# Tile 2's scores one step later, half of VectorE's score work behind the gate, VectorE's weight behind the powers, layer two's odd rows later

## The reference

```python
for t in range(S):                      # recurrence
    m_new = np.maximum(f_gate[:, :, t] + m, i_gate[:, :, t])
    f_stab = np.exp(f_gate[:, :, t] + m - m_new)
    i_stab = np.exp(i_gate[:, :, t] - m_new)
    C = f_stab * C + i_stab * outer(v_t, k_t)
    n = f_stab * n + i_stab * k_t
    y_t = sigmoid(o_gate_t) * (C @ q_t) / np.maximum(np.abs(n @ q_t), 1.0)
xn = x / np.sqrt(np.mean(x * x, axis=-1, keepdims=True) + 1e-06) * rms_g   # layer one
g = xn @ w_gate
x1 = (g * sigmoid(g) * (xn @ w_val)) @ w_out
h = x1 @ w_in                                                              # layer two
out = np.maximum(0.01 * h, h) @ w_out2
```

## Time and profile before

| | us |
|---|---|
| median of 3 runs | 453.7 (451.58 to 454.03) |
| the profiled execution | 453.02 |
| its span | 451.2 |
| TensorE busy | 428.3, 95% of the span |
| VectorE busy | 233.6, 52% |
| ScalarE busy | 196.0, 43% |
| GpSimd busy | 91.3, 20% |
| granted TensorE clock, mean | 0.989 of 2.4 GHz |

### The profile page before, as it was taken

How to read it: one execution, slowest core, us unless ns; L and a number is a source line. 1 busy time by engine, 2 the same in 40 slices (tenths; PEclk the granted TensorE clock), 3 DMA queues, 4 the chain that set the end, 5 groups by cost and what they waited for, 6 DMA issues and landing times.

```text
span 451.2 us, 8148 instructions
## 1 busy us (share of the span) xinstructions
PE 428.3 (95%) x3202; PEld 377.0 (84%) x3202; DVE 233.6 (52%) x439; ACT 196.0 (43%) x431; POOL 91.3 (20%) x92
## 2 busy tenths in 40 slices
PE   2768999899999999999999999999999999999997
PEld 1658998899888888888888888899999999999996
DVE  7754767567648565554633435533343433444534
ACT  1873775356527344323433225454343343333332
POOL 1473974222111111100433101440000000000000
PEclk9986999999999999999999999999999999999999
DMA  6886381333303050000222200410000000010101
GB/s 181 288 278 203 125 267 50 121 122 121 103 20 92 30 172 1 0 1 0 65 64 65 64 0 4 127 34 0 1 0 1 0 2 0 1 58 1 58 1 58
DMA packets 10756, 31.37 MB, mean 70 GB/s; under 512 B 1328, under 2 KB 3088, under 8 KB 10720
## 3 DMA queue, kind: packets, MB, share of 16 engines
q1 hardware_dynamic: 10720, 30.87, 21.2%
HBM read 28.85 MB, written 2.02 MB: 68 GB/s over the span
## 4 chain that ended last, share of the span: by engine, by line
PE 82%; issue 6%; POOL 4%; ACT 3%; DVE 2%; DMA 2%; POOLq 0%; DVEq 0%; ACTq 0%
PE gate_ps L1017 23%; PE value_ps L1017 23%; PE out_ps L1054 9%; PE out_ps L1090 9%; PE turn_ps L1090 6%; PE out_ps L1058 3%; PE c_ps L1090 3%; PE turn_ps L992 2%; POOL w_sb L422 2%; PE turn_ps L953 2%; ACT expo L485 1%; PE turn_ps L970 1%; DMA expo<-decay_scratch 1%; POOL ms L399 1%; POOL expo L391 1%
## 5 line engine op out<-in xcount | busy, mean ns | idle before, releaser
L1017 PE MATMUL gate_ps<-x_hi,w_sb 128*128 128x512 f32 (+1 forms) x280 | 69.0, 369 | 3.8 <-DVE act_buf L800 2.3
L1017 PE MATMUL value_ps<-x_hi,w_sb 128*128 128x512 f32 (+1 forms) x280 | 69.7, 372 | 0.0
L558 ACT ACTIVATE h_hi<-hid 128x512 fp32r<-128x512 f32 (+1 forms) x46 | 24.7, 537 | 76.2 <-DVE hid L806 76.1
L1017 PEld LDWEIGHTS gate_ps<-x_hi,w_sb 128*128 128x128 f32 x280 | 47.4, 191 | 12.3 <-issue 2.7
L1017 PEld LDWEIGHTS value_ps<-x_hi,w_sb 128*128 128x128 f32 x280 | 47.7, 193 | 6.2
L825 DVE TENSOR_TENSOR h_lo<-hid,h_hi 128x512 fp32r<-128x512 f32 x48 | 33.2, 693 | 33.7 <-ACT h_hi L563 33.7
L800 DVE SCALAR_TENSOR_TENSOR act_buf<-act_buf,gate_ps 128x512 f32<-128x512 f32 (+1 forms) x46 | 26.1, 568 | 46.6 <-ACT act_buf L544 46.6
L1054 PE MATMUL out_ps<-h_hi,w_sb 128*128 128x512 f32 (+1 forms) x184 | 47.8, 346 | 0.0
L563 ACT ACTIVATE h_hi<-hid 128x512 fp32r<-128x512 f32 x48 | 30.3, 632 | 38.3 <-DVE hid L813 37.2
L544 ACT ACTIVATE act_buf<-gate_ps 128x512 f32<-128x512 f32 (+1 forms) x46 | 23.0, 500 | 48.4 <-PE gate_ps L1017 48.2
L820 DVE TENSOR_TENSOR h_lo<-hid,h_hi 128x512 fp32r<-128x512 f32 (+1 forms) x46 | 32.5, 708 | 22.1 <-ACT h_hi L558 21.8
(11 more groups left out here) (140 smaller groups left out, 774.0 us busy)
## 6 DMA issues: line engine op xcount, KB each, us to landing
raw<-in_w SPq DMA_DIRECT2D x12, 544.0 KB, 4.5
expo<-decay_scratch SPq DMA_DIRECT2D x12, 512.0 KB, 5.4
att_sb<-in_tok SPq DMA_DIRECT2D x12, 484.0 KB, 4.7
raw<-in_w SPq DMA_DIRECT2D x16, 352.0 KB, 3.0
att_sb<-in_qk SPq DMA_DIRECT2D x24, 160.0 KB
out_y<-y_acc SPq DMA_DIRECT2D x12, 160.0 KB, 1.9
consts_sb<-in_consts SPq DMA_DIRECT2D x1, 129.5 KB, 2.3
gates_sb<-in_gates SPq DMA_DIRECT2D x1, 96.0 KB, 2.4
```

What stands on the lines that cost most here:

```text
L558: nc.scalar.activation(h_hi[:, r, cols], hid[:, r, 0:width(s)], ACT.Copy).then_inc(hi_done, 1)
L1017: last = nc.tensor.matmul(ps[:, 0:n], lhs, rhs, start=(j == 0), stop=(j == len(xs) - 1))
```

## The change

1. `BESIDE` changes for tiles 2, 3 and 4. Tile 2: S, R and O one step later. Tile 3: T one step earlier. Tile 4: R and O one step earlier. With that tile 2 and tile 3 become "at once".
2. VectorE does `scores(n, 1)` behind `gated(s)` in place of ahead of it.
3. The high part of tile 0 (`x_high(0)`) moves from ScalarE to VectorE as `first_x_high`, with a semaphore of its own; both first_state calls stand ahead of it. VectorE's `lo_first` of weight block 1 moves behind x_low(1).
4. ScalarE does `high1(0)` ahead of hi_weights(3), and only half of tile 2's decays ahead of step 1; the rest comes behind tanh(1).
5. GpSimd: weigh_keys(3) ahead of inverse_rms(2), and fade_state(4) ahead of lo_weights(11).
6. In layer two `x2_odd(2)` moves from behind step 47 to behind step 53, and the loop is cut in two there.

```diff
-BESIDE = {2: (0, 1, 2, 4), 3: (3, 5, 6, 8), 4: (7, 9, 10, 11), 5: (10, 12, 13, 14), 6: (14, 15, 16, 17),
+BESIDE = {2: (1, 2, 3, 4), 3: (3, 5, 6, 7), 4: (7, 8, 9, 11), 5: (10, 12, 13, 14), 6: (14, 15, 16, 17),
...
             lo_weights(5)
+            weigh_keys(3)
             inverse_rms(2)
-            weigh_keys(3)
             lo_weights(6)
...
             exponents(5)
+            fade_state(4)
             lo_weights(11)
-            fade_state(4)
...
             square(1)
-            x_high(0)
             normalise(1)
             x_high(1)
             hi_weights(2)
             first1(0, width(0))
+            high1(0)
             hi_weights(3)
-            for z in range(2):
-                decay(2, z)
-            keep_last(2)
-            high1(0)
+            for n in beside(1)["S"]:
+                decay(n, 0)
...
+            def first_x_high():
+                dve.wait_ge(consts_in, 16)
+                dve.wait_ge(t_done, 1)
+                for k in range(2):
+                    nc.vector.tensor_scalar(x_hi[:, k, 0:P], turned_ps(0)[:, k * P:(k + 1) * P], rms_sb[:, k:k + 1],
+                                            None, ALU.mult)
+                nc.vector.tensor_scalar(x_odd[0:ODD, 0:P], turned_ps(0)[0:ODD, 2 * P:3 * P], rms_sb[0:ODD, 2:3],
+                                        None, ALU.mult).then_inc(first_xhi, 1)
...
             first_state(0)
+            first_state(1)
+            first_x_high()
+            x_low(0)
+            x_low(1)
+
             lo_first(DVE_W)
-            x_low(0)
-            first_state(1)
-            x_low(1)
...
                 for n in work["S"]:
                     scores(n, 0)
-                    scores(n, 1)
                 for n in work["O"]:
                     denominator(n)
                 if s < STEPS1:
                     gated(s, width(s))
+                for n in work["S"]:
+                    scores(n, 1)
...
             step2(STEPS1 + 1)
+            steps2(STEPS1 + RING, STEPS1 + GF)
+
             x2_odd(CHUNKS - 1)
-            steps2(STEPS1 + RING, STEPS1 + (CHUNKS + 1) * GF)
+            steps2(STEPS1 + GF, STEPS1 + (CHUNKS + 1) * GF)
...
-            pe.wait_ge(xhi_done, FIRST)
+            pe.wait_ge(first_xhi, 1)
+            pe.wait_ge(xhi_done, FIRST - 1)
             gate(0)
```

More of the change, by code:

```diff
@@ L234, in build @@
         t_done = sem("t_done")
+        first_xhi = sem("first_xhi")
         xhi_done = sem("xhi_done")
@@ L517, in x_high @@
                 act.wait_ge(t_done, n + 1)
-                if n == 0:
+                if n == 1:
                     act.wait_ge(consts_in, 16)
@@ L781, in finish @@
                     .then_inc(y_done, 1)
+            def first_x_high():
[6 more added lines that the diff above has]
+                                        None, ALU.mult).then_inc(first_xhi, 1)
             def x_low(n):
-                dve.wait_ge(xhi_done, n + 1)
+                if n:
+                    dve.wait_ge(xhi_done, n)
+                else:
+                    dve.wait_ge(first_xhi, 1)
                 tok = slice(n * P, (n + 1) * P)
```

## The result

| | before | after |
|---|---|---|
| median, us (20 executions each) | 452.56 (451.16 to 454.45) | 450.35 (449.27 to 451.54) |
| profiled execution, us | 453.02 | 449.81 |
| its span, us | 451.2 | 448.0 |

The account below looks back on a forecast made before the run. TensorE was taken to set the time, so only its waits and low clock could be won. Gains of 9.5 less new losses of 5.05 gave net 4.5, from 453.0 or 453.7 to 448.5 or 449.2; forecast 449.0 us, range 445.5 to 452.0.

Parts of the forecast that it names:

- the 1.2 that I had called the forecast: Whole kernel: time within 1.2 us of the forecast 449.0, given a chance of 0.48.
- gate(2)'s wait: Step 2, tile 2's scores a step later: 2.2 us won, new loss 0.85, net 1.35.
- tile 2's turn: Step 5, first transposes of tile 2, by tile 4's pattern in before: a new wait, 1.6 us lost.
- tile 3's: Tile 3's turn a step earlier: its power stands behind weight 9 on GpSimd; 1.8 us lost, 1.1 gained.
- from_state(4): It now waits for x_low(3), which is behind high weight 10 and x_high: another 0.35 us lost.
- layer two: x2_odd moved: the 0.7 us wait at layer two's start goes, 0.3 lost at the new place.
- weight 1 behind x_low(1) costs 0: VectorE's subtraction comes ahead of GpSimd's weight 2 by 0.15 us and ends in time for gated(0): cost 0.
- the clock, 3.1: gate(2) to gate(3): without the 2 us wait TensorE stays at 2.4 GHz; gain 3.1 us, between 0 and 3.3.
- ahead of step 0, 0.75: Tile 1's second power on GpSimd ends 0.94 earlier with weight 1 moved away; counted as 0.75 us won.
- tiles 3 and 4: Moves of tiles 3 and 4: 1.8 + 0.35 lost, 1.1 + 1.65 won, net 0.6 us won.
- GpSimd gets in first: Rival at weight 2: VectorE's subtraction ends at 30.4, gate(1) starts 2.3 us late; 451.3 to 454.5, chance 0.08.
- The clock falls at a new wait: Rival: one fall at tile 2's or 3's turn, costing 1.7 to 3.3 us; 450.7 to 452.3, chance 0.16.

Follow-up runs that it names:

- a_lock: The changed kernel with GpSimd waiting for VectorE's low part of weight 1 before it begins weight 2; 448.69 us, ratio to before 0.9915.
- b_fill: The kernel before with 16 idle products on TensorE between value(1) and gate(2), filling the 2 us wait; 451.48 us against 452.76, ratio 0.9983.
- a_w1_early: The changed kernel with VectorE's subtraction of weight 1 back behind first_state(0); 449.76 us, ratio to before 0.9932.
- a_scores_front: The changed kernel with both halves of VectorE's scores ahead of gated again; 450.26 us, ratio to before 0.9956.

## Why the prediction was right and wrong

**Right.** The direction, the range, and the places of the waits in each part but one. That 450.35 lies only 1.35 above 449.0 is in part luck: the forecast started from a median of three runs, 453.7, and the median of twenty is 452.56. It lies just outside the 1.2 that I had called the forecast, and for none of the rivals' reasons alone. gate(2)'s wait went from 2.04 to 0.57, tile 2's turn waits 1.45 (I had copied 1.45 from tile 4), tile 3's 1.40 (forecast 1.6), tile 4's none, from_state(4) 0.17, layer two 0.2. Copying the chain of tile 4 to tile 2 by its pattern of the table was the best step of the forecast.

**Wrong: weight 1 behind x_low(1) costs 0.** It costs 1.3 by the runs of a_lock beside the changed kernel (0.8 in the traced pair, 1.6 over all executions). I had said that whoever is first makes the other wait, and had looked for who is first: VectorE was, by 0.11 us. What I missed is that `lo_first` is two instructions, and that GpSimd, waiting, gets in between them. The rows of before could have told it: the slow power ended at 24.28, and 0.55 earlier, at 23.73, is the end of VectorE's first subtraction (22.64 + 1.22 = 23.86), to 0.1, and not of the second, which comes behind it. I read it as having waited through both. The page of the Trainium skill that I weighed, "SBUF — State Buffer", section "Who interferes with whom", says of VectorE's two-port modes that whoever issues first gets the shared ports for the whole instruction, and of an instruction with two SBUF inputs that it contends with GpSimd's reads. The trace agrees that one waits for the other's whole instruction, and instruction is the word that matters: here nothing was held from one to the next.

**Wrong in size: the clock, 3.1.** In the pair of profiled executions it is right (2.9 by b_fill). For the median it is 0.8 to 1.3, as if only some executions of before paid it. I made the sum against one profiled execution with the fall and then laid it on a median of three runs, two of which lie in the upper group. This is the largest miss of the forecast: 1.8 to 2.3.

It also hides what the later scores are worth by themselves. From gate(0) to gate(6) before takes 27.4 (26.42 to 53.81), the changed kernel 25.8 (26.51 to 52.34), a_lock 25.0 and b_fill 24.9 (26.91 to 51.85), with its wait of 2 us still in place and filled. So where the clock stays up, moving tile 2's pieces a step later wins nothing in these steps, and with the lock loses 0.9: its gain is the clock's. The forecast's terms say the same (2.2 less 0.85 and 1.6 is a loss of 0.25), though it did not say so. Tile 2 put back alone was not run.

**Wrong in size: ahead of step 0, 0.75.** The power is quicker by 0.93, but in the profiled pair nothing of it is left at gate(0), for the two reasons given above. a_w1_early, whose power starts at 23.37 like the changed kernel's at 23.40, has its transposes 1.0 later (25.59 against 24.60). So the term is right between like executions, and the forecast was made from one in which this stretch had the higher clock.

**Too low: tiles 3 and 4.** 1.1 to 1.4 in place of 0.6.

The sum anew, for the profiled pair and by stretches. Up to gate(0) 0.75 was forecast, and 0.1 was lost. From gate(0) to gate(6) 2.85 was forecast (2.2 and 3.1, less 0.85 and 1.6) and 1.55 came; of the 1.3 missing 0.8 is the lock (25.8 against 25.0), 0.2 the clock, and 0.3 stays open. From gate(6) to gate(13) it was 0.45 and 1.1, behind it 0.4 and 0.6. Together 4.45 was forecast and 3.2 measured. For the medians no such account by stretches can be made. Taking parts of the change back gives 1.1 for tiles 3 and 4, 0.8 for layer two and nothing for weight 1 and the power together. That leaves some 0.3 of the 2.2 for tile 2 with its clock, where 2.85 was forecast, all with an error of half a microsecond or more. With the lock mended, a_lock has 448.7, where the forecast's sum for the profiled execution gave 448.5. This agreement is luck: a_lock lies 2.9 to 4.1 below the medians of before beside it, not 4.5, and the sum was laid on an execution of before above those medians.

**The rivals.** "GpSimd gets in first" was the nearest to the truth, with 0.08 of the chance: its place was right. Of its 2.3, gated(0) was 1.75 late (30.89, where a_lock has 29.14) and gate(1) 1.25 (31.44 against 30.19). That 28.9 and 2.3 is 31.2, close to 31.44, is luck, since gate(0) came 1.0 later than forecast; and the clock did not add to it. "The clock falls at a new wait" was seen in one trace, of a_scores_front, at a price of 1.5. The prediction put the point at which a wait brings the clock down between 1.45 and 2.04. The traces do not bear that out: 1.41 brought it down in one, and 1.59 left it up in another, so the length of the wait alone does not decide. How often the clock falls in the changed kernel stays open, as only two of its executions were traced.

## What to carry to other kernels

VectorE and GpSimd held each other up in the places shown, where both subtracted with two inputs from SBUF, and a pair of such instructions was not one block: the other engine started between them. So order the two engines by a semaphore, or let the long neighbour wait, when one of the pair is on the critical path. When a stretch at low clock lies behind a wait, look at the spread of the times before costing it: two groups of times may mean that it is paid in a part of the executions only, and one profile shows one execution of one group. Price the change without the clock as well, to see what is left of it. A chain that binds can be read off a place where the same pattern of the schedule already stands; here the wait read off so (1.45) came out as 1.45.

## What the runs showed that I had not expected

- VectorE's 0.22 us subtraction took 2.38 with a GpSimd instruction ahead of it that takes 2.37 by itself (a_lock), although VectorE's list had no gap between its two subtractions.
- The granted clock reads 1.00 ahead of the first recorded change, even where four products of 256 columns take 1.20 in place of 0.71. The mean of 0.999 for the changed kernel says nothing of its first 30 us.
- A wait of 1.40 to 1.59 us at the turn of tile 2 or 3 left the clock up in every trace but one, and in that one a wait of 1.41 brought it down. The Trainium skill, "TensorE: Matmul & The Clock Gate", section "What's actually happening", says that the chip's look at TensorE's work runs freely and does not begin anew with a kernel, so that the point of a change differs from run to run. That would fit the two groups of times and the one fall, and no run here shows it by itself.
